# Gate logits of four FFN blocks: from TensorE transposes and products to VectorE multiply-and-sum instructions

## The reference

```python
def _moe_ref(x, w_in, w_out):            # 2304 x 512, inner size 2048
    h = x @ w_in
    sp = np.where(h > 20.0, h, np.log1p(np.exp(np.minimum(h, 20.0))))
    g = h * np.tanh(sp)
    return (g @ w_out).astype(np.float32)

def _moe2_ref(x, modality_id, w_gate, modality_bias, w1, w2):
    logits = x @ w_gate + modality_bias[modality_id]     # 2304 x 8
    e_idx = np.argmax(logits, axis=1)
    ...
    gate_w = probs[np.arange(N), e_idx]
    for e in range(E):
        mask = e_idx == e
        h = np.maximum(x[mask] @ w1[e], 0.0)
        out[mask] = gate_w[mask, None] * (h @ w2[e])
```

## Time and profile before

| | before |
|---|---|
| median of 3 runs | 932.55 us (932.0 to 933.66) |
| profiled execution, its own time | 932.91 us |
| its span | 931.1 us |
| mean granted TensorE clock | 0.964 |
| TensorE busy | 860.2 us (92%) |
| VectorE busy | 506.2 us (54%) |
| ScalarE busy | 429.5 us (46%) |
| GpSimd busy | 232.5 us (25%) |
| DMA, mean over the span | 55 GB/s |

### The profile page before, as it was taken

How to read it: one execution, slowest core, us unless ns; L and a number is a source line. 1 busy time by engine, 2 the same in 40 slices (tenths; PEclk the granted TensorE clock), 3 DMA queues, 4 the chain that set the end, 5 groups by cost and what they waited for, 6 DMA issues and landing times.

```text
span 931.1 us, 16050 instructions
## 1 busy us (share of the span) xinstructions
PE 860.2 (92%) x4845; PEld 733.0 (79%) x4846; DVE 506.2 (54%) x1023; ACT 429.5 (46%) x1186; POOL 232.5 (25%) x218
## 2 busy tenths in 40 slices
PE   5888888879999999999999999997699999999995
PEld 3666667758998998988998998986578888888883
DVE  6899999944665555555555555576762111111110
ACT  3777777764555445445345345454043222222221
POOL 1567776543211001001001002053311111111110
PEclk9799999978999999999999999999799999999998
DMA  5555555221000000000000000220061111111100
GB/s 108 148 148 143 150 147 149 72 56 45 26 22 35 1 1 34 0 0 34 0 0 34 0 0 34 91 91 0 34 219 42 45 45 37 40 45 45 45 34 13
DMA packets 88197, 51.57 MB, mean 55 GB/s; under 512 B 64480, under 2 KB 77280, under 8 KB 88160
## 3 DMA queue, kind: packets, MB, share of 16 engines
q1 hardware_dynamic: 85040, 41.16, 15.8%
q0 software_dynamic: 3120, 9.96, 3.2%
HBM read 41.67 MB, written 9.70 MB: 55 GB/s over the span
## 4 chain that ended last, share of the span: by engine, by line
PE 72%; DVE 16%; issue 5%; ACT 2%; DMA 2%; POOL 1%; DVEq 1%; SPq 0%; ACTq 0%; POOLq 0%
PE ps L1440 8%; PE ps L1442 8%; PE ps L1441 8%; PE ps L1330 7%; PE ps L1331 7%; PE ps L1332 7%; PE ps L1306 6%; PE ps L1305 6%; PE ps L1311 6%; DVE ssum L903 3%; DVE smax L893 3%; DVE kdz L878 2%; DMA vwin<-in_v_dram 2%; PE ps L1463 2%; PE ps L1347 1%
## 5 line engine op out<-in xcount | busy, mean ns | idle before, releaser
L992 DVE TENSOR_SCALAR Tb<-Eb 128x384 f32<-128x384 f32 x96 | 41.4, 431 | 133.9 <-ACT Eb L737 133.9
L737 ACT ACTIVATE Eb<-ps 128x384 f32<-128x384 f32 x96 | 47.1, 491 | 141.5 <-PE ps L1311 141.3
L667 ACT ACTIVATE prob<-ps,nmax 96x111 f32<-96x111 f32 (+1 forms) x256 | 87.7, 355 | 23.7 <-DVE nmax L897 23.4
L1306 PE MATMUL ps<-xh,WA 128*128 128x384 f32 x288 | 98.2, 341 | 0.0
L1305 PE MATMUL ps<-xh,WA 128*128 128x384 f32 x288 | 97.7, 339 | 0.0
L562 POOL TENSOR_TENSOR xl<-xT,xh 128x384 fp32r<-128x384 f32 x24 | 26.8, 1144 | 280.4 <-ACT xh L709 280.4
L1330 PE MATMUL ps<-WA,gh 128*128 128x512 f32 x216 | 87.1, 403 | 2.4 <-DVE gl L951 2.4
L1332 PE MATMUL ps<-WA,gl 128*128 128x512 f32 x216 | 85.4, 395 | 0.0
L1331 PE MATMUL ps<-WA,gh 128*128 128x512 f32 x216 | 85.2, 394 | 0.0
L746 ACT ACTIVATE Rb<-Tb 128x384 f32<-128x384 f32 x96 | 50.5, 526 | 73.5 <-DVE Tb L994 73.5
L1171 DVE TENSOR_TENSOR hTl<-ps,hTh 128x1024 fp32r<-128x1024 f32 x19 | 23.2, 1223 | 97.5 <-ACT hTh L800 97.5
(11 more groups left out here) (218 smaller groups left out, 2030.8 us busy)
## 6 DMA issues: line engine op xcount, KB each, us to landing
wsraw<-in_moe_w_dram SPq DMA_DIRECT2D x32, 256.0 KB, 3.3
vwin<-in_v_dram SPq DMA_DIRECT2D x32, 166.5 KB
qraw<-in_q_dram SPq DMA_DIRECT2D x32, 144.0 KB, 3.0
kraw<-in_k_dram SPq DMA_DIRECT2D x32, 144.0 KB, 3.0
vdraw<-in_v_dram SPq DMA_DIRECT2D x32, 144.0 KB
y_rows<-yrow SPq DMA_DIRECT2D x6, 768.0 KB, 3.6
wraw<-in_moe_w_in_dram SPq DMA_DIRECT2D x12, 256.0 KB, 5.6
wraw<-in_moe_w_out_dram SPq DMA_DIRECT2D x12, 256.0 KB, 3.4
```

What stands on the lines that cost most here:

```text
L667: last = act.activation(prob[0:np_, a.s6, n * w:(n + 1) * w], ps[0:np_, o:o + w], ACT.Exp, scale=sc, bias=nmax[0:np_, a.s6, n:n + 1], accu ...
L1306: pe.matmul(dst, lo, xh[:, kk, :], start=False, stop=False)
```

## The change

**What it does.** Block 0's gate, made in block 1, and block 5's stay on TensorE (`PE_GATES` = 1). For blocks 1 to 4 the transposes, the copies to `yT` and the small products are gone. In their place VectorE multiplies a row tile of `yrow` (128 x 512) by the gate weights of one expert and sums along the row, one `scalar_tensor_tensor` with `accum_out` for each tile and expert. The product goes to bank 7, the sum to one column of `lg`. That is 24 instructions a block. `gate_piece` places two into each iteration from j = 4 to 15: one between n and g, one behind g. After eight of them the bias is added (`gate_bias`).

The instruction needs the weights on every partition. SP loads the 4 x 1024 values of `w_gate`, repeated on all 128 partitions, into the first 1024 columns of each of x's four chunks, which blocks 0 to 2 have used up. The load waits for `x_lo` of block 2 and stands between the stores of blocks 1 and 2. The weights of one expert lie eight floats apart there. The space that follows the FFN (`wsraw`, routing tables) is laid out anew around these columns. ScalarE's `y_evac` waits for `logit_out` in place of `y_turned`.

```diff
+        FIRST_DVE_GATE = 3
+        PE_GATES = FIRST_DVE_GATE - 2
...
+            def load_gate():
+
+                sp.wait_ge(x_lo, FIRST_DVE_GATE * NK)
+                for kk in range(NK):
+                    sp.dma_start(xT[:, kk * N:kk * N + GW],
+                                 w_gate[kk * P:(kk + 1) * P, :].rearrange("(o p) e -> o (p e)", o=1).broadcast_to([P, GW])
+                                 ).then_inc(wg_all, 16)
+
+            for i in range(FIRST_DVE_GATE - 1):
                 store_rows(i)
+            load_gate()
+            with sp.Fori(FIRST_DVE_GATE - 1, NTB - 1) as i:
+                store_rows(i)
...
-                wait(act, y_turned, i * NS)
+                wait(act, logit_out, i * NS)
...
+            def gate_row(q, s, e):
+
+                qn = q * NS + s
+                wait(dve, logit_sum, (q - PE_GATES) * NS * E + s * E + e)
+                if e == 0:
+                    wait(dve, y_out, qn + 1)
+                wg_e = xT[:, :].rearrange("p (kk n) -> p kk n", kk=NK)[:, :, 0:GW].rearrange(
+                    "p kk (d e) -> p kk d e", e=E)[:, :, :, e]
+                dve.scalar_tensor_tensor(
+                    out=bank(7).rearrange("p (kk d) -> p kk d", kk=NK), in0=yrow[:, s, :].rearrange("p (kk d) -> p kk d", kk=NK),
+                    scalar=1.0, in1=wg_e, op0=ALU.mult, op1=ALU.mult, accum_out=lg[:, ds(qn * E + e, 1)]
+                ).then_inc(logit_sum, 1)
+
+            def gate_bias(q, s):
+                qn = q * NS + s
+                dve.wait_ge(logit_sum, (q - PE_GATES) * NS * E + (s + 1) * E)
+                dve.tensor_tensor(lg[:, ds(qn * E, E)], lg[:, ds(qn * E, E)], bia[:, ds(qn * E, E)], ALU.add
+                                  ).then_inc(logit_out, 1)
+
+            GATE_FROM, GATE_EACH = 4, 2
+
+            def gate_piece(before, j, n):
+
+                if before is None or isinstance(before, int) and before < PE_GATES or j < GATE_FROM:
+                    return
+                w = (j - GATE_FROM) * GATE_EACH + n
+                if isinstance(before, int) and before == PE_GATES and w == 0:
+                    dve.wait_ge(wg_all, 16 * NK)
+                if w and w % E == 0:
+                    gate_bias(before, w // E - 1)
+                gate_row(before, w // E, w % E)
+                if w == NS * E - 1:
+                    gate_bias(before, NS - 1)
...
                     dve.tensor_tensor(Ec, Tc, hc, ALU.mult).then_inc(n_done, 1)
+                    gate_piece(before, j, 0)
                     dve.wait_ge(n_done, c + 1)
                     dve.wait_ge(r_done, c + 1)
                     dve.tensor_tensor(Ec, Ec, Rc, ALU.mult).then_inc(g_done, 1)
...
-                    if before is not None:
+                    if isinstance(before, int) and before < PE_GATES:
                         if j in (2, 4, 6):
                             gate_copy(before * NS + j // 2 - 1)
                         if j in (3, 5, 7):
                             gate_out(before * NS + j // 2 - 1)
-
+                    gate_piece(before, j, 1)
```

More of the change, by code:

```diff
@@ L142, in build @@
         NES = NC2
[L143 to L156, removed]
@@ L180, in build, with __init__, tensor, close @@
[L180 to L183, removed]
+        GW = P * E
+        RAW = 2 * DM
+        class Region:
+            def __init__(self, name, floats):
+                self.name, self.left = name, 4 * floats
+            def tensor(self, name, shape, dt=F32):
+                n = 1
+                for d_ in shape[1:]:
+                    n *= d_
+                self.left -= (n * (2 if dt == BF16 else 4) + 31) // 32 * 32
+                assert self.left >= 0, (name, self.left)
+                return alloc(ctx, name, shape, dt)
+            def close(self):
+                if self.left:
+                    alloc(ctx, self.name + "_rest", [P, self.left // 4])
@@ new lines, in build @@
+        wsraw = []
+        R = Region("space1a", GW)
+        rA = R.tensor("rA", [P, NTOK, E])
+        rB = R.tensor("rB", [P, NTOK, E])
+        rC = R.tensor("rC", [P, NTOK, E])
+        oh = R.tensor("oh", [P, NTOK, E], BF16)
+        r18 = R.tensor("r18", [P, 8, NTOK])
+        i18 = R.tensor("i18", [P, 3, NTOK], I32)
+        e8 = R.tensor("e8", [P, 12, E])
+        e8i = R.tensor("e8i", [P, 3, E], I32)
+        gparts = R.tensor("gparts", [P, 3, NTOK], BF16)
+        grest = R.tensor("grest", [P, 2, NTOK])
@@ new lines, in build @@
+        slotf = R.tensor("slotf", [P, 2, NSX])
+        gate = R.tensor("gate", [P, NSX])
+        gidx = R.tensor("gidx", [P, NSX], I32)
+        R.close()
+        wsraw.append(alloc(ctx, "wsraw0", [P, RAW]))
+        R = Region("space1b", N - RAW)
+        iot_i = R.tensor("iot_i", [P, NI], I32)
+        assert 4 * NI <= 4 * (N - GW - RAW)
+        iot = R.tensor("iot", [P, NI])
+        tcmp = R.tensor("tcmp", [P, 2, NSX, E])
+        e64 = R.tensor("e64", [P, 6, E, E])
+        tabf = R.tensor("tabf", [P, 4, NSX])
@@ new lines, in build @@
+        sidx = R.tensor("sidx", [P, NSX], I32)
+        R.close()
+        wsraw.append(alloc(ctx, "wsraw1", [P, RAW]))
+        R = Region("space1c", N - RAW)
+        tri = R.tensor("tri", [P, P], BF16)
+        ones = R.tensor("ones", [P, P], BF16)
+        selp = R.tensor("selp", [P, NTOK, P], BF16)
+        R.close()
+        wsraw.append(alloc(ctx, "wsraw2", [P, RAW]))
+        R = Region("space1d", N - RAW)
+        tab_i = R.tensor("tab_i", [P, 2, NSX], I32)
+        tab_off = R.tensor("tab_off", [P, NSX], I32)
@@ L184, in build @@
+        tab_need = R.tensor("tab_need", [P, NSX], I32)
+        tab_next = R.tensor("tab_next", [P, NSX], I32)
+        tab_buf = R.tensor("tab_buf", [P, NSX], I32)
+        tab_expert = R.tensor("tab_expert", [P, E], I32)
+        tab_n = R.tensor("tab_n", [P, 3], I32)
+        R.close()
+        wsraw.append(alloc(ctx, "wsraw3", [P, RAW]))
+        alloc(ctx, "space1e", [P, N - GW - RAW])
+        assert len(wsraw) == NRAW == NK
         WD = alloc(ctx, "WD", [P, NF * SLAB], F32R)
@@ L584, in _ @@
                 for which in range(2):
-                    last = pool.tensor_tensor(e_part(c, which, 1), wsraw[:, c % NRAW, which * DM:(which + 1) * DM],
+                    last = pool.tensor_tensor(e_part(c, which, 1), wsraw[c % NRAW][:, which * DM:(which + 1) * DM],
                                               e_part(c, which, 0).bitcast(F32), ALU.subtract)
@@ L723, in expert_hi @@
                 for which in range(2):
-                    last = act.copy(e_part(buf + c, which, 0), wsraw[:, c % NRAW, which * DM:(which + 1) * DM])
+                    last = act.copy(e_part(buf + c, which, 0), wsraw[c % NRAW][:, which * DM:(which + 1) * DM])
                 last.then_inc(ws_hi, 1)
@@ L1009, in ffn_block @@
                             gate_out(before * NS + j // 2 - 1)
+                    gate_piece(before, j, 1)
+            assert (NF - GATE_FROM) * GATE_EACH == NS * E
             ffn_block(0, None)
-            with dve.Fori(1, NTB - 1) as i:
+            for i in range(1, FIRST_DVE_GATE):
+                ffn_block(i, i - 1)
+            with dve.Fori(FIRST_DVE_GATE, NTB - 1) as i:
                 ffn_block(i, i - 1)
@@ L1179, in next_expert @@
                         last = dve.tensor_tensor(
-                            e_part(buf + c, which, 1), wsraw[:, c % NRAW, which * DM:(which + 1) * DM],
+                            e_part(buf + c, which, 1), wsraw[c % NRAW][:, which * DM:(which + 1) * DM],
                             e_part(buf + c, which, 0).bitcast(F32), ALU.subtract)
@@ L1350, in ffn_block @@
             def ffn_block(i, before):
+                gated = before is not None and before < PE_GATES
                 for j in range(2, NF):
                     ffn_in(i, j)
-                    if before is not None and j in (2, 4, 6):
+                    if gated and j in (2, 4, 6):
                         gate_turn(before * NS + j // 2 - 1, j // 2 - 1)
-                    if before is not None and j in (3, 5, 7):
+                    if gated and j in (3, 5, 7):
                         gate_mm(before * NS + j // 2 - 1)
@@ L1366, in _ @@
             ffn_block(0, None)
-            with pe.Fori(1, NTB - 1) as i:
-                ffn_block(i, i - 1)
-            ffn_block(NTB - 1, NTB - 2)
+            for i in range(PE_GATES):
+                ffn_block(i + 1, i)
+            with pe.Fori(PE_GATES + 1, NTB - 1) as i:
+                ffn_block(i, None)
+            ffn_block(NTB - 1, None)
             pe.wait_ge(first_expert, 1)
```

32 lines of the change are left out of this document (5 added, 27 removed).

## The result

| | before | changed |
|---|---|---|
| median | 933.05 us (4 runs, 932.0 to 933.66) | 948.78 us (4 runs, 946.45 to 950.43) |
| profiled execution: span | 931.1 us | 944.7 us |
| mean granted TensorE clock | 0.964 | 0.955 |

The changed kernel is slower: 1.0172 times the time before, 95% interval 1.0157 to 1.0188. That is 15.7 us by the medians, where the prediction had 12.8. A second set of runs on another chip gave 950.87 us against 932.86, 18.0 us more and a ratio of 1.0178 (1.0145 to 1.0211). The profiled execution of the changed kernel was the fastest of its four (946.45 us).

What follows compares the result with a forecast made beforehand. TensorE was taken to bound blocks 1 to 4, VectorE and GpSimd the last block's later part. Terms -15.6 + 9.6 + 6.3 + 1.2 + 10.3 + 1.0 = +12.8 us on the 931.1 span gave 943.9, hence 945.3 us; range 926 to 972.

Steps and rivals of the forecast that it cites:

- The bound and the saving: FFN blocks 1 to 4: TensorE bounds in program order; twelve tiles leave it at 1.30 us each, saving 15.6 us.
- The price d: VectorE time of one new instruction to the next start: 1.1 us chosen; range 1.0 to 1.2 given chance 0.45.
- The block ends: Ends of blocks 2 to 4: VectorE's built-up delay and meeting GpSimd stall TensorE; net 1.4 us more a block.
- the two terms for lateness and xl: Blocks 2 to 4: 3.2 us a block from VectorE's delay in steps 4 to 14, 2.1 from meeting GpSimd's xl tiles.
- The term of 2.1: Step 15 of blocks 2 to 4: two new instructions between xl tiles or before gl(14), 2.1 us a block, 6.3 together.
- The last block: Last FFN block to the first product behind it: slower steps, longer periods and a lower clock, net 8.6 us more.
- The seven periods: Last block, j = 9 to 15: VectorE and GpSimd taking turns lengthen each period from 5.30 to 6.77 us, 10.3 together.
- The load: Gate weights on SP's queue behind the second store: all there by about 373, cost 0, at most 3 us if late.
- Case (a): Rival on VectorE's stepped read: it costs nothing, d = 0.68, only GpSimd collisions remain, -7.1 us, 925.4 us; chance 0.17.
- Case (b): Rival on VectorE's stepped read: as slow as the GpSimd row or slower, d = 1.3, +32.6 us, 965; chance 0.28.
- Case (c): Rival on VectorE's stepped read: rate in between, d = 1.03, +6.2 us, 938.8 us; no chance of its own given.
- Case (d): Rival on the weight load: weights land late, one VectorE stall of up to 3 us atop any case; no chance given.

Runs made afterwards that it cites:

- the forms measured alone: Kernel before plus 36 extra VectorE instructions at its end, three of each form; only durations read: 0.70 us at step 2, 1.08 us for the stepped form.
- The idle products: Changed kernel plus 18 unread TensorE products at the ends of blocks 2 to 4, during the wait for gl: 944.77 us, against 950.87 for the changed kernel beside it.
- the expert-major kernel: Changed kernel with gate weights laid out expert by expert, so the new instruction reads without a step: 922.14 us, 0.9887 times the kernel before.

## Why the prediction was right

**The bound and the saving** were read rightly. With the weights expert by expert and nothing late at the block's end, blocks 3 and 4 take 67.7 us in place of 71.7: 4.0 a block, where 3 x 1.30 = 3.9 were counted from the earlier trace rows.

**The price d**, on which all else hung, was set at 1.1 us between 0.68 and 1.30. It is 1.06 to 1.12 from start to start, and a step of VectorE took 4.42 to 4.60 us where 4.48 was worked out. Its parts were off: the sum costs 0.01 and not 0.08 (0.61 beside the 0.60 of the earlier trace rows), and the stepped read 0.45 to 0.5 and not 0.42. The choice between the bounds was a judgement, and that it came out so near is in part luck; only the forms measured alone have settled it.

**The block ends** were under-counted, 1.4 us a block against 1.8, 2.9 and 3.0. The missing term is the clock. I had it at the end of the last block, where the earlier trace rows shows it behind a wait of 2.92 us, but not at the three block ends, although my own sum put about as long a stall there. The idle products price it at 0.9, 2.3 and 2.4 us. Without it a block costs 72.5 - 67.7 = 4.8 us over its work, and the two terms for lateness and xl had 3.2 + 2.1 = 5.3. The term of 2.1 had nearly the right size for a wrong reason. I had the two new instructions of step 15 between the xl tiles or in front of gl(14). They stand behind gl(14) (496.19), and no x-low product waits for GpSimd at these block ends. It is VectorE's own lateness that pushes the two instructions ahead of them into GpSimd's tiles, 1.48 us, and 3.2 + 1.48 is close to the 4.8. The x-low products wait only in the expert-major kernel, 0.70 us each time.

**The last block** came out at +9.1 against +8.6, and that is luck: its terms are off in both directions and cancel. The steps up to 8 gave back only 0.5 us of the 2.7 expected (3.9 saved less 1.2). The collision starts a step earlier (the end of SCALAR_TENSOR_TENSOR of step 8 comes 6.65 us behind that of step 7, 5.58 before), and the first 12 products of the block, still at the low clock of block 4's end, take 2.93 us in place of 2.24. The seven periods of 6.6 us, not 6.77, add 9.2 and not 10.3, and what stands behind them adds 0.3 and not 1.0, although TensorE's wait there grew from 2.92 to 4.21 us. The order was also another than I had it: GpSimd is there first and the second new instruction waits, 2.27 us long. The sum of turns is nearly the same.

**The load** landed in time. The first new instruction starts at 371.48 with no wait ahead of it, 8 us behind the last of the four issues (363.5), whose transfers took up to 7.9 us. There was nothing to spare.

**The rivals.** Case (a), a step without a price, is what the expert-major kernel runs: 922.1 measured, 925.4 from the sum, since the collisions cost 0.85 and 0.25 a step and not 1.3 and 0.63. So the sum also holds, within 3.3 us, for the form that the change doesn't have. Case (b) didn't come: no form tried took more than 1.09 us alone. Case (c) had d = 1.03 and 938.8 us; the price in the kernel lies a little above it, and the clock term, which it lacks as well, makes up most of the rest. Case (d) didn't come.

**The total** owes some of its nearness to chance. 15.7 us were measured and 12.8 worked out. The FFN parts by themselves rose by 16.8 us in the profiled execution, and the untouched rest was 3.2 us shorter in it. On the second chip the medians are 18.0 us apart. The sum was thus low by 3 to 5 us: the clock at the three block ends was left out (0.9 + 2.3 + 2.4 = 5.6), and the other terms together had somewhat too much.

## What to carry to other kernels

Moving work from the engine that bounds a stage to an idle one pays only if the free time per step holds it at its real price, and an operand's step in SBUF can raise that price (here from 0.61 to 1.1 us); laying data out once, in the order in which it is read, turned this change from a loss into a gain. Ask not only whether an engine has room on average but where its lateness comes due: the same instructions two steps earlier cost 13 us less. Where a stall of some 3 us appears on TensorE, count the half-speed products behind it as a term of their own.

## What the runs showed of the hardware

- VectorE reads a float source at full rate with a step of 1 or 2 floats (0.70 us for 512 elements), slower at 3 (0.84), and at one lower rate from 4 to 8 (1.07 to 1.08). Only steps of the second source were tried.
- `accum_out` adds next to nothing where the next instruction doesn't wait for it: its read-out has a row of 0.14 us, but the next instruction starts with it (459.87 for both), and 0.61 us from start to start stand beside 0.60 without a sum. Where the next one waited, and the product went to PSUM, it added 0.07 us.
- GpSimd and VectorE take turns on whole instructions: TENSOR_SCALAR of 0.36 us takes 1.43 beside a split, a new instruction of 1.19 takes 2.27, and each split waits in its turn. Line 1073, with one source in SBUF and one in PSUM, kept its 0.54 us beside the xl tiles (495.73, while they run from 493.10 to 498.50).
- TensorE's clock went from 2.4 to 1.2 GHz during a wait of 3.54 us and stayed there for nearly 7 us, at the end of block 2 after a wait of 3.56 us for only some 3. Why the two differ stays open. Behind the 0.85 us waits of the last block before, products kept their 0.23 us. In the longer periods of the changed kernel's last block some out groups ran at 0.43 us a product (those from 634.65 and 647.92 on) and others, of the same period, at 0.23 (from 621.37, 628.00 and 641.21 on). It cost nothing there, since VectorE and GpSimd set the period; why one group was slowed and not the next stays open.
